# Transposes ahead of the value products in each turn of a head pair, in an fp32 attention and two-layer kernel on one core

## The reference

```python
def _attn_ref(q, k, v, proj):                      # q, k, v: (2, 8, 768, 64), proj: (64, 6)
    q_bits = (np.einsum('bhsd,dk->bhsk', q, proj) > 0).astype(np.int64)
    k_bits = (np.einsum('bhsd,dk->bhsk', k, proj) > 0).astype(np.int64)
    powers = 2 ** np.arange(n_bits)
    q_bucket, k_bucket = np.sum(q_bits * powers, axis=-1), np.sum(k_bits * powers, axis=-1)
    mask = q_bucket[:, :, :, None] == k_bucket[:, :, None, :]
    scores = scale * np.matmul(q, k.transpose(0, 1, 3, 2))
    scores = np.where(mask, scores, -1000000000.0)
    scores = scores - np.max(scores, axis=-1, keepdims=True)
    attn = np.exp(scores)
    attn = attn / (np.sum(attn, axis=-1, keepdims=True) + 1e-09)
    return np.matmul(attn, v).astype(np.float32)
...
x = attn_out.transpose(0, 2, 1, 3).reshape(1536, 512)
h = x @ w_in;  g = np.where(h >= 1, h, np.where(h <= -1, 0.0, (h + 1) ** 2 / 4));  x = g @ w_out
h = x @ w2_in; g = h - np.tanh(h);                                                 return g @ w2_out
```

## Time and profile before

| | us |
|---|---|
| median of 3 runs (lowest to highest) | 761.44 (761.32 to 761.51) |
| the profiled execution | 761.38 |
| its span, first to last instruction | 759.6 |
| TensorE busy | 751.2 (99%) |
| VectorE busy | 426.4 (56%) |
| ScalarE busy | 343.4 (45%) |
| GpSimd busy | 290.3 (38%) |
| attention, first scores to the last turn's scores | 6.5 to 222.4 |

### The profile page before, as it was taken

The page is one execution under the profiler, slowest core; times in us unless marked ns, Lnnn a source line. Parts: engine busy times, 40 slices in busy tenths (PEclk is TensorE's granted clock), DMA queues, the critical chain, the costliest instruction groups (busy, mean ns, idle before and its releaser), DMA issues.

```text
span 759.6 us, 11673 instructions
## 1 busy us (share of the span) xinstructions
PE 751.2 (99%) x3726; PEld 637.8 (84%) x3726; DVE 426.4 (56%) x741; ACT 343.4 (45%) x679; POOL 290.3 (38%) x226
## 2 busy tenths in 40 slices
PE   7999999999999999999999999999999999999998
PEld 5989989988998888888888888888888888888886
DVE  6999999999995674344333677762221322232223
ACT  6888888888893323343333423241211321222122
POOL 7677977877989991000000466650000000000000
PEclk9999999999999999999999999999999999999999
DMA  6544454454324231000000123210000100010001
GB/s 238 154 129 140 135 129 133 137 141 119 109 77 149 81 113 57 1 0 1 1 0 1 56 83 111 84 55 1 1 0 1 55 0 0 0 55 1 1 0 56
DMA packets 21032, 49.48 MB, mean 65 GB/s; under 512 B 4782, under 2 KB 6958, under 8 KB 21002
## 3 DMA queue, kind: packets, MB, share of 16 engines
q1 hardware_dynamic: 20858, 48.68, 21.2%
q10 hardware_dynamic: 144, 0.39, 0.1%
HBM read 41.26 MB, written 3.19 MB: 59 GB/s over the span
## 4 chain that ended last, share of the span: by engine, by line
PE 86%; DVE 8%; ACT 3%; issue 2%; DMA 0%; DVEq 0%; ACTq 0%
PE ps L684 29%; PE ps L603 29%; PE ps L594 9%; PE ps L580 9%; DVE g_raw L920 5%; PE ps L560 4%; PE ps L567 4%; PE ps L517 2%; DVE g_mid L917 1%; ACT g_hi L794 1%; ACT g_mid L788 1%; DMA qk_raw<-qk 0%; DVE clamped L843 0%; DVE g_lo L928 0%; DVE q_b L828 0%
## 5 line engine op out<-in xcount | busy, mean ns | idle before, releaser
L603 PE MATMUL ps<-x_hi,w 128*128 128x512 f32 (+1 forms) x768 | 251.9, 389 | 0.0
L928 DVE TENSOR_TENSOR g_lo<-g_raw,g_hi 128x512 fp32r<-128x512 f32 x96 | 72.1, 751 | 243.2 <-ACT g_hi L794 243.2
L794 ACT ACTIVATE g_hi<-g_raw 128x512 fp32r<-128x512 f32 x96 | 60.7, 632 | 288.1 <-PE ps L684 224.6
L603 PEld LDWEIGHTS ps<-x_hi,w 128*128 128x128 f32 x768 | 144.1, 188 | 29.7
L603 PE MATMUL ps<-x_lo,w 128*128 128x512 f32 (+1 forms) x384 | 149.4, 389 | 0.0
L684 PE MATMUL ps<-g_hi,w 128*128 128x512 f32 x384 | 125.9, 389 | 0.3 <-DVE g_lo L928 0.3
L684 PE MATMUL ps<-w,g_hi 128*128 128x512 f32 x384 | 118.1, 389 | 0.0
L860 DVE TENSOR_TENSOR p_lo<-ps,p_hi 128x384 fp32r<-128x384 f32 x192 | 97.9, 551 | 11.6 <-ACT p_hi L740 11.2
L376 POOL TENSOR_SCALAR w<-stage 128x1024 fp32r<-128x1024 f32 x32 | 37.4, 1167 | 164.1 <-PE ps L684 162.1
L740 ACT ACTIVATE p_hi<-ps 128x384 fp32r<-128x384 f32 x192 | 84.4, 489 | 29.7 <-PE ps L580 28.2
L730 ACT ACTIVATE probs<-clamped,row_stats 128x768 f32<-128x768 f32 x96 | 89.7, 934 | 5.6 <-DVE clamped L843 5.1
(11 more groups left out here) (64 smaller groups left out, 859.4 us busy)
## 6 DMA issues: line engine op xcount, KB each, us to landing
stage<-weights SPq DMA_DIRECT2D x32, 512.0 KB, 3.3
qk_raw<-qk SPq DMA_DIRECT2D x15, 384.0 KB, 3.6
q_raw<-qq SPq DMA_DIRECT2D x15, 384.0 KB, 4.0
k_raw<-kk SPq DMA_DIRECT2D x15, 384.0 KB, 5.0
v_raw<-v SPq DMA_DIRECT2D x16, 192.0 KB, 4.0
inv_wide<-factors SPq DMA_DIRECT2D x16, 192.0 KB, 4.6
out<-stage SPq DMA_DIRECT2D x12, 256.0 KB, 2.1
q_a<-q_b SPq DMA_DIRECT2D x14, 192.0 KB
```

Of the source, the lines that this page charges most:

```text
L603: last = nc.tensor.matmul(ps[:, f % H_BANKS, :], w[:, f, wp, k * P:(k + 1) * P], xs[:, k, bass.ds(t * TOK, TOK)], start=(k == 0 and wp == ...
L794: nc.scalar.activation(g_hi[:, slot, :], g_raw[:, slot, :], ACT.Copy).then_inc(g_hi_ready, 1)
L928: nc.vector.tensor_tensor(g_lo[:, slot, :], g_raw[:, slot, :], g_hi[:, slot, :].bitcast(F32), ALU.subtract).then_inc(g_split, 1)
```

## The change

In every turn outside the drain, the transposes of tile n-4 are issued directly behind the scores of tile n, and the value products of tile n-8 behind the transposes. The drain keeps its order. Nothing is added or taken away, and the programs of the other engines stay as they are.

```diff
                 for n in range(PT_TILES):
                     if not drain:
                         scores(p, n)
-                    old = trailing(p, n, PV_LAG)
-                    if old and not (drain and n >= PV_LAG):
-                        weighted_values(*old)
+                    older, old = trailing(p, n, PV_LAG), trailing(p, n, TRANSPOSE_LAG)
+                    if old and not drain:
+                        transposes(*old)
+                    if older and not (drain and n >= PV_LAG):
+                        weighted_values(*older)
                     if drain:
                         early_hidden(n)
-                    old = trailing(p, n, TRANSPOSE_LAG)
-                    if old and not (drain and n >= TRANSPOSE_LAG):
+                    if drain and n < TRANSPOSE_LAG:
                         transposes(*old)
```

## The result

The changed kernel takes **787.47 us** (median; 787.40 to 787.61 in 4 runs), the kernel before 761.48 (761.32 to 761.56) beside it. The ratio is 1.034 with an interval of 1.0328 to 1.0352: 26.0 us slower. The prediction was 784.3 in 779 to 790. The profiled execution has a span of 785.7 us where it had 759.6.

The account below looks back on a forecast made before the run. TensorE sets the pace, VectorE 5% behind. A pair goes from 28.0 to 27.3 + 2.5 (buffer's wait) + 1.26 (knock-on) = 31.0 us; over all pairs 761.4 + 22.9 = 784.3 us, range 779.0 to 790.0.

Parts of the forecast that it names:

- The mechanism and its price: Turns 2, 5, 11: `p_hi` copy waits for value products; transposes 0.64 late, block 0.19 longer, 0.83 us per turn.
- the fourth stall: Turn 8: no such loss, since the bit products behind turn 7 put 1.29 us in between.
- The knock-on: Late turns 0, 3, 4, 9 and 10 behind the stalls, with VectorE full: 1.26 us per pair.
- The sum: Whole attention: pairs 1 to 5 +15.0, pair 6 +3.2, pair 7 +3.9, pair 0 +0.8; +22.9 us.
- The branch: TensorE's loop end: 0.22 us bubble hidden by value products behind the transposes, five times, a gain of 1.1 us.
- The new neighbours: TensorE's blocks in new order: cost 0, with 0.03 us per turn either way, 3 us over 88 turns.
- (a): Only the first-order loss, no knock-on: 779.4 us; chance 0.10 with what lies between 775 and 780.
- (b): Faster: the copy to `p_hi` released earlier, only gains left, up to 4.6 us, 756.8; chance 0.04.
- (c): No change: copy's wait doesn't bind and today's waits stay, 760.3 us, inside 0.2%; chance 0.03.
- (d): TensorE's pauses cost clock: half clock in one turn of four adds 45 us, 829; chance 0.01.
- (e): More knock-on: each of three hand-overs costs 0.05 us more, 7.1 in all, 791.4; chance 0.10 with above.

Follow-up runs that it names:

- experiment 5: Changed kernel with VectorE's clamp on half the columns: 780.73 us; kernel before with the same: 758.65; changed kernel with ScalarE's exponent halved besides: 776.96.
- (4): Changed kernel with FACTOR_LAG = 9 in place of 8, so VectorE's inverts stand in turns 3 and 9, not 2 and 8: 784.52 us.
- experiment 6: Kernel before with TensorE's loop over pairs 1 to 6 written out, so no branch between pairs: 760.93 us, ratio 0.9992.
- experiment 2: Changed kernel with the old order, value products ahead of transposes, in turns 1, 4, 7 and 10 alone: 775.63 us.
- the last of 6: Kernel before (old order) with PV_LAG = 7, all value products one turn earlier: 795.51 us.

## Why the prediction was right, and where its terms were off

*The mechanism and its price* held to 0.01 us in turn 2 of pair 3: from the value products' end 0.03 to the copy, 0.49, 0.03, `p_lo` 0.55, 0.06 to the transposes, 0.64 late and 0.19 for the block. Turns 2 and 11 are 0.83 too long, turns 5 and 6 together 0.84, turns 7 and 8 together 0.00: the bit products do hide the fourth stall.

*The knock-on* is the term that was too small: 1.26 per pair predicted, 1.66 measured.

| turn | extra us, predicted | measured | what the runs showed |
|---|---|---|---|
| 0 and 3 | 0.22 each | 0.27 each | ScalarE too, with VectorE at the same time (5) |
| 4 and 10 | 0.23 each | 0.24 each | VectorE with an invert (4) |
| 9 | 0.36 | 0.63 | the fold priced from another turn |

In turns 0 and 3 I had named VectorE alone. Both engines come to the same time there (in the changed kernel the copy ahead of turn 3's `p_lo` ends at 102.57 and VectorE is free from the clamp at 102.61), and experiment 5 shows that the turns stay at 2.33 with VectorE relieved. That VectorE alone would hold them up is not shown. So that part of the sum came near by luck.

The missing 0.05 is in the size of the block. A block that was held up takes 0.19 more, as in the price of 0.83; the knock-on sums count 0.14 of it. In turn 3 of pair 3 the transposes start at 103.21 where 103.14 was due, 0.07 late, and take 1.01: 0.27 in all. In turns 4 and 10 the same omission hardly shows, since the transposes are 0.04 late there and not 0.09.

For turn 9 the trace after shows the term:

```profile
116.17 1.02 DVE L861 TENSOR_TENSOR p_lo<-ps,p_hi 128x384 fp32r<-128x384 f32 x2 [0.97 <-ACT p_hi L741]
...
117.22 0.55 DVE L872 TENSOR_TENSOR x_pair<-ps,low 64x384 f32<-64x384 f32 x1
...
117.80 0.67 DVE L822 TENSOR_SCALAR bits<-ps,mask_s 72x384 fp32r<-72x384 f32 x1
...
119.27 1.01 DVE L861 TENSOR_TENSOR p_lo<-ps,p_hi 128x384 fp32r<-128x384 f32 x2
...
119.87 1.01 PE L580 MATMUL ps<-ident,probs 128*128 128x128 f32 x6 [0.28 <-DVE p_lo L861]
```

From one first `p_lo` to the next it is 3.10 us, where I had 0.94 + 0.47 + 0.58 + 0.88 = 2.87. This 0.23 and the 0.05 of the block make up the excess of 0.27. Two smaller errors cancel: this chain starts 2.86 us into turn 7 and not 2.79, as the copy starts 0.09 behind the value products there, and the transposes start 0.05 behind `p_lo` where the sum had 0.12, twice what its row gives. The fold starts 1.05 behind the first `p_lo`, not 0.94, and is followed by the threshold after 0.58, not 0.47. I had taken the fold's price from turn 1. It is not what comes behind the fold that makes the difference, but which fold it is: those of turns 10 and 1 (groups 0 and 1) write partitions 0 to 63 of `x_pair`, those of turns 4 and 7 (groups 2 and 3) partitions 64 to 127. Over all pairs, before and after, the first kind starts 0.93 to 0.99 behind the first `p_lo` and is followed after 0.46 to 0.50; the second kind starts 1.04 to 1.06 behind it and is followed after 0.58 to 0.59, by a clamp just as by a threshold (99.42 and 100.00 in turn 4 of the kernel before). The kernel before has turn 7's instructions at the higher price too:

```profile
105.89 1.02 DVE L860 TENSOR_TENSOR p_lo<-ps,p_hi 128x384 fp32r<-128x384 f32 x2 [0.17 <-ACT p_hi L740]
106.95 0.55 DVE L871 TENSOR_TENSOR x_pair<-ps,low 64x384 f32<-64x384 f32 x1
107.53 0.67 DVE L821 TENSOR_SCALAR bits<-ps,mask_s 72x384 fp32r<-72x384 f32 x1
```

*The sum.* Pairs 1 to 5 grew by 3.39 to 3.48 us each, 17.2 (predicted 15.0), pair 6 by 3.7 (3.2), pair 7 with its last turn by 4.3 (3.9), pair 0 by 0.7 (0.8). Another 0.4 of the 26.1 us of span lies ahead of the first scores, which start at 6.86 us instead of 6.47; the second ones are only 0.14 later (8.82 for 8.68), so most of it comes back within pair 0. In the traces of the other kernels here that start is anywhere between 6.4 and 7.6, so I don't count it to the change. From the first matmul of the two layers (251.44 after, 225.25 before) to the end it is 534.3 us in both kernels: the layers are as long as before, as predicted.

*The branch.* "issue" ahead of a pair's first scores is gone: pairs 5 and 6 both end with a turn 11 of 2.89. But the gain of 1.1 is an upper bound, since experiment 6 shows that 0.09 of the 0.22 comes back as a longer turn 0 when nothing else is in the way.

*The new neighbours* cost nothing: in the undisturbed turn 1 the time is 2.06 in either order.

*The rivals.* (a) would have needed the knock-on to vanish; it was larger. (b) and (c) fell with the first row of waits. (d): the clock stayed at 1.00 in the stretch above, where TensorE pauses for 0.5 to 0.8 us in three turns of twelve. The Trainium skill (TensorE: Matmul & The Clock Gate, psum-queue depth-cycling) reports a swing between the two levels in another kernel with frequent short pauses; this trace has such pauses and no swing. (e) is the direction in which the time came out, by another way than it named: the hand-overs were mostly as in the rows; the fold of turn 7 and the held-up blocks cost more than counted.

## What to carry to other kernels

Before two blocks are swapped on an engine that issues in order, list what each block releases, not only what it waits for: here the value products freed a buffer that another engine was about to write, and the wait for it, never late before, became the slowest event of three turns in twelve. A double buffer's distance is counted from the last read to the next write, and it can be lost by moving the read as well as the write. Where two engines come within 0.1 us of the same time behind such a stall, as VectorE and ScalarE in turns 0 and 3, price both of them, and take the price of an instruction from the very turn that it stands in.

## What was not expected of the hardware

TensorE, ScalarE and VectorE mostly hand over in 0.03 to 0.06 us (0.09 behind the value products of turn 7, 0.12 in experiment 2, 0.23 in the last of 6), so a chain over three engines is nearly the sum of its instructions, and the one of the result could be priced to 0.01 us beforehand. A loop's branch left TensorE short of work for 0.22 us, with 0.33 us of queued matmuls ahead of it, and for nothing with 1.04 us ahead. A VectorE instruction of the same shape was followed by the next after 0.47 or after 0.58 us. The longer time goes with folds that write the upper 64 partitions, between instructions that write from partition 0 on; in the pairs of both traces every such fold has it and no other does. No run moved a fold's output to test it.
